# Turning q one tick later in a fused attention and two-MLP kernel, and reordering the last step of its second MLP

## The reference

```
out_d = sm_attn(q_d, k_d, v_d)          # pooled by 4
attn  = softmax(where(|i-j|<4, scale*q@k.T, -1e9))
x     = repeat(out_d, 4) + attn@v       # 2304 x 512
x     = (s*relu(x @ w_in)**2 + b) @ w_out        # 512 -> 2048 -> 512
out   = ((x @ w_a) * (x @ w_b)) @ w_out2         # 512 -> 1536 -> 512
```

## Time and profile before

| | |
|---|---|
| median of three runs | 975.58 us |
| the profiled execution | 975.64 us, of which the span of the trace is 973.8 us |
| PE busy | 951.3 us, 98% of the span |
| ACT, DVE, POOL busy | 474.5, 611.1, 202.0 us |
| granted clock of PE, mean | 0.984 |
| DMA | 71.41 MB, 73 GB/s on average |

### The profile page before, as it was taken

One profiled execution on the slowest core, in us unless ns is written; L12 is line 12 of the kernel. 1 busy time (PEld: TensorE's weight loads), 2 busy tenths in 40 slices (PEclk: granted clock), 3 DMA queues, 4 the chain that ended last, 5 costly groups with the idle time before them and its releaser, 6 DMA issues.

```text
span 973.8 us, 18322 instructions
## 1 busy us (share of the span) xinstructions
PE 951.3 (98%) x6902; PEld 898.5 (92%) x6902; DVE 611.1 (63%) x1087; ACT 474.5 (49%) x1112; POOL 202.0 (21%) x216
## 2 busy tenths in 40 slices
PE   6899999999999999999999999999999999999997
PEld 5799999999999999999999999999999999999996
DVE  5788655655555556555547666666856667766642
ACT  4677554545554445454434544444634345644432
POOL 2200211001210011200012033333333333333310
PEclk8599999999999999999999999999999999999999
DMA  8346220111300122101041142222442222422201
GB/s 199 104 136 164 65 59 20 45 45 43 88 21 20 48 64 67 44 19 44 14 154 34 50 137 66 66 66 66 135 143 79 67 66 66 130 66 65 75 24 66
DMA packets 129352, 71.41 MB, mean 73 GB/s; under 512 B 63248, under 2 KB 120304, under 8 KB 129264
## 3 DMA queue, kind: packets, MB, share of 16 engines
q1 hardware_dynamic: 128224, 69.94, 25.0%
q10 hardware_dynamic: 1040, 0.29, 0.1%
HBM read 60.76 MB, written 9.44 MB: 72 GB/s over the span
## 4 chain that ended last, share of the span: by engine, by line
PE 88%; ACT 6%; DVE 3%; issue 2%; DMA 1%; SPq 1%; POOL 0%; ACTq 0%; DVEq 0%
PE bank L736 27%; PE bank L686 19%; PE bank L672 18%; PE bank L752 15%; ACT sml L795 3%; PE bank L572 2%; PE bank L636 2%; PE bank L619 1%; PE bank L629 1%; PE bank L548 1%; DMA natk<-in_k 1%; ACT smp L786 1%; PE bank L603 1%; PE bank L566 1%; ACT kT L774 1%
## 5 line engine op out<-in xcount | busy, mean ns | idle before, releaser
L736 PE MATMUL bank<-wx 128*128 128x384 f32 x1512 | 287.4, 336 | 0.6 <-ACT u L977 0.6
L736 PEld LDWEIGHTS bank<-wx 128*128 128x128 f32 x1512 | 267.1, 188 | 14.6 <-ACT u L977 0.9
L686 PE MATMUL bank<-g_hi,wx 128*128 128x288 f32 x1024 | 232.1, 302 | 0.0
L672 PE MATMUL bank<-wx 128*128 128x288 f32 x1536 | 226.9, 296 | 0.5 <-ACT relu L889 0.5
L672 PEld LDWEIGHTS bank<-wx 128*128 128x128 f32 x1536 | 211.7, 189 | 0.7 <-ACT relu L889 0.7
L1236 POOL TENSOR_TENSOR raw<-raw 128x256 f32<-128x256 f32 x144 | 143.3, 1013 | 302.9 <-DVE wx L1156 263.4
L686 PEld LDWEIGHTS bank<-g_hi,wx 128*128 128x128 f32 x1024 | 171.4, 188 | 5.3 <-issue 5.2
L752 PE MATMUL bank<-wx 128*128 128x512 f32 x648 | 173.4, 394 | 0.8 <-DVE wx L1156 0.8
L686 PE MATMUL bank<-g_lo,wx 128*128 128x288 f32 x512 | 151.5, 296 | 0.0
L752 PEld LDWEIGHTS bank<-wx 128*128 128x128 f32 x648 | 119.3, 188 | 17.2 <-DVE wx L1156 1.5
L1112 DVE SCALAR_TENSOR_TENSOR g_lo<-relu,b_col,g_hi 128x288 fp32r<-128x288 f32 x128 | 70.6, 552 | 80.4 <-ACT g_hi L894 80.4
(11 more groups left out here) (70 smaller groups left out, 858.8 us busy)
## 6 DMA issues: line engine op xcount, KB each, us to landing
raw<-in_moe_w_b SPq DMA_DIRECT2D x72, 128.0 KB, 2.3
raw<-in_moe_w_a SPq DMA_DIRECT2D x72, 128.0 KB, 2.3
raw<-in_moe_w_out SPq DMA_DIRECT2D x36, 256.0 KB, 2.8
vnat<-in_v SPq DMA_DIRECT2D x32, 144.0 KB
o_transposed<-o_sb SPq DMA_DIRECT2D x8, 576.0 KB, 3.4
o_raw<-o_transposed SPq DMA_DIRECT2D x6, 768.0 KB, 6.3
out<-y SPq DMA_DIRECT2D x18, 256.0 KB, 2.3
natq<-in_q SPq DMA_DIRECT2D x63, 72.0 KB, 2.1
```

Source lines behind the costliest of these rows:

```text
L672: mm = nc.tensor.matmul(HB[:, 0:HALF], wi(w, kd, f), xs(x, c % 2)[:, kd], start=(kd == 0 and j == 0), stop=(kd == KD - 1 and j == 2))
L686: mm = nc.tensor.matmul(ACC[o][:, 0:HALF], wo(w, f, o), g[:, slot % GB, :], start=(f == 0 and j == 0), stop=(f == F1 - 1 and j == 2))
L736: mm = nc.tensor.matmul(dst, left(w, n, a, kd), right(x, i)[:, kd * HC:(kd + 1) * HC], start=(opens and kd == 0 and m == 0), stop=(kd == K ...
```

## The change

Two edits, which share nothing.

1. For units from 4 on, `turn_q`, `take_q` and `sum_q` stand one tick later: -3, -3 and -2 in place of -4, -4 and -3. On PE the three transposes of q move from between up and down of a slot to behind that down, ahead of the next up. On ACT the copy of qT moves from behind relu (L889) to behind the high part of g (L894) and, in the first 16 slots, behind the weight splits (L851). The boot ticks of units 0 to 3 stay.
2. In the last of the 36 steps the products run in the order 0, 1, 2, 4, 5, 3, 6 with the previous step's `down_2` placed anew between them, and DVE has an order of its own: prod0, then c22, then the low part of prod0, then c12, prod1 and its low part.

```diff
--- before.py
+++ after.py
@@ -52,6 +52,10 @@
 N7 = len(PRODUCTS)
 LEFT_AT = {"a11": 0, "a12": 1, "a22": 2, "s1": 3, "s2": 4, "s3": 5, "s4": 6}
 PIECES = 3
+
+SECONDS = (), (0,), (1,), (2, 3), (4, 5), (), ()
+LAST_ORDER = 0, 1, 2, 4, 5, 3, 6
+LAST_SECONDS = (), (0,), (1, 2), (5,), (3, 4), (), ()
 BLK1 = KD * P + DM
 BLK2 = N7 * LEFT + DM
 PIECE = BLK2 // PIECES
@@ -642,7 +646,7 @@
                 for u in at_tick(g, 0, -5, TURN_SKEW):
                     if leads(u):
                         turn_k(u)
-                for u in at_tick(g, 1, -4, TURN_SKEW):
+                for u in at_tick(g, 1, -3, TURN_SKEW):
                     turn_q(u)
                 for u in at_tick(g, 13, 8):
                     if not alone(u):
@@ -757,10 +761,11 @@
                     mm.then_inc(p_used, 1)
 
             for n in range(STEPS):
-                for i in range(N7):
+
+                for i in range(N7) if n < STEPS - 1 else LAST_ORDER:
                     product(n, i)
                     if n > 0:
-                        for tt in ((), (0,), (1,), (2, 3), (4, 5), (), ())[i]:
+                        for tt in (SECONDS if n < STEPS - 1 else LAST_SECONDS)[i]:
                             down_2(n - 1, tt)
             for tt in range(TT):
                 down_2(STEPS - 1, tt)
@@ -972,7 +977,7 @@
                 if over:
                     for tt in range(3):
                         take_y(c - 1, tt)
-                act.wait_ge(up_done, N7 * n + 5)
+                act.wait_ge(up_done, N7 * n + (5 if n < STEPS - 1 else 4))
                 past(act, c22_ready, n)
                 nc.scalar.activation(u3_sb, X_BANK, ACT.Copy).then_inc(u3_taken, 1)
                 if over:
@@ -1075,7 +1080,7 @@
                 for u in at_tick(g, 1, -4, TURN_SKEW):
                     if leads(u):
                         sum_k(u)
-                for u in at_tick(g, 2, -3, TURN_SKEW):
+                for u in at_tick(g, 2, -2, TURN_SKEW):
                     sum_q(u)
 
             def split_w_lo(f):
@@ -1156,6 +1161,23 @@
                 nc.vector.tensor_tensor(p_lo[:, n % 2, h], prod[h], p_hi[:, n % 2, h].bitcast(f32), ALU.subtract)\
                   .then_inc(pl_ready, 1)
 
+            def last_products():
+                n = STEPS - 1
+                dve.wait_ge(up_done, N7 * n + 5)
+                dve.wait_ge(c11_ready, n + 1)
+                nc.vector.tensor_tensor(prod[0], X_BANK, c11_sb, ALU.mult).then_inc(pr1_ready, 1)
+                dve.wait_ge(u3_taken, n + 1)
+                dve.wait_ge(up_done, N7 * n + 6)
+                nc.vector.tensor_tensor(c22_sb, Y_BANK, u3_sb, ALU.add).then_inc(c22_ready, 1)
+                split_product_lo(n, 0)
+                dve.wait_ge(up_done, N7 * n + 7)
+                dve.wait_ge(u2_taken, n + 1)
+                nc.vector.tensor_tensor(c12_sb, Y_BANK, u2_sb, ALU.add).then_inc(c12_ready, 1)
+                dve.wait_ge(c12_ready, n + 1)
+                dve.wait_ge(c22_ready, n + 1)
+                nc.vector.tensor_tensor(prod[1], c12_sb, c22_sb, ALU.mult).then_inc(pr2_ready, 1)
+                split_product_lo(n, 1)
+
             for n in range(STEPS):
                 c, f = divmod(n, F2)
                 renew = f == F2 - 1 and c + 1 < NC2
@@ -1181,6 +1203,9 @@
                     split_w2_lo(n + 2, 1)
                 if 4 <= f < 8 and c + 1 < NC2:
                     right_sum(c + 1, f - 4)
+                if n == STEPS - 1:
+                    last_products()
+                    break
                 dve.wait_ge(u3_taken, n + 1)
                 nc.vector.tensor_tensor(c22_sb, Y_BANK, u3_sb, ALU.add).then_inc(c22_ready, 1)
                 if renew:
@@ -1188,14 +1213,10 @@
                 dve.wait_ge(up_done, N7 * n + 6)
                 dve.wait_ge(c11_ready, n + 1)
                 nc.vector.tensor_tensor(prod[0], X_BANK, c11_sb, ALU.mult).then_inc(pr1_ready, 1)
-
-                if n == STEPS - 1:
-                    split_product_lo(n, 0)
                 dve.wait_ge(up_done, N7 * n + 7)
                 dve.wait_ge(u2_taken, n + 1)
                 nc.vector.tensor_tensor(c12_sb, Y_BANK, u2_sb, ALU.add).then_inc(c12_ready, 1)
-                if n < STEPS - 1:
-                    split_product_lo(n, 0)
+                split_product_lo(n, 0)
                 dve.wait_ge(c12_ready, n + 1)
                 dve.wait_ge(c22_ready, n + 1)
                 nc.vector.tensor_tensor(prod[1], c12_sb, c22_sb, ALU.mult).then_inc(pr2_ready, 1)
```

## The result

The changed kernel takes 986.68 us in the median of four runs (986.18 to 987.52), the kernel before 975.38 (974.59 to 975.60). The profiled execution took 987.52 us, with a span of 985.7 against 973.8.

The account below looks back on a forecast made before the run. PE was taken to bound the kernel, with 88% of the chain. The terms -4.2 + 5.2 + 4.7 + 1.2 + 1.0 - 0.5 = +7.4 us on 975.64 gave 983.0 us, range 980.5 to 985.5.

Parts of the forecast that it names:

- 11 leading units: Units with a k turn: turn_q no longer waits for the copy of kT, 0.38 us each, -4.2 us.
- 12 units without a k turn: From unit 12 on, turn_local waits 0.43 us each for the later copy of q, +5.2 us.
- units 6, 7: ACT's copy of q stands behind two weight splits, so PE waits 2.35 us in each, +4.7 us.
- unit 8: A leading unit whose copy of q also stands behind weight splits; PE waits, +1.2 us.
- the boot's end: Unit 4's later sum of q delays its scores and mask, then unit 5's copy comes later: +1.0 us.
- the last step: c12 starts 0.6 us earlier, product 6 waits 0.14 for c22: -0.5 us.
- what takes the stall's place: turn_local may start 0.94 us behind g_hi's start: leading units wait 0, units without a k turn 0.43 us.
- rival 1: Clock falls at the new stalls, 2.0 us lost per fall: one gives 985.0 us, two 987.0; chance 0.18.
- Rival 2: Copy of q reaches turn_local in time, so 5.2 + 4.7 + 1.2 is not lost: 971.9 us; chance 0.04.

Follow-up runs that it names:

- e6: Changed kernel with unit 4's copy and sum of q back at their old ticks: 985.32 us against 975.74 for the kernel before.
- e7: Kernel before, with q turned, copied and summed later only for the 12 units without a k turn from unit 12 on, plus new last step: 981.11 us.
- e4: Changed kernel with ACT's copy and DVE's sum of q back where they stood, only PE's turn later: 971.44 us against 975.63 for the kernel before.
- e10: Kernel before with only the tick of PE's turn of q changed, old last step: 972.11 us against 975.79.
- e3: Changed kernel with ACT copying q ahead of the two weight splits in the first 16 slots: 978.51 us against 975.63 for the kernel before.
- e1: Kernel before with only the last step's new order: 975.69 us against 975.63.
- e9: Changed kernel with 20, 20 and 15 extra unread matmuls ahead of turn_local for units 6, 7, 8: 983.76 us against 975.79 for the kernel before.
- e2: Kernel before with only q turned, copied and summed one tick later, old last step: 987.14 us against 975.63.
- e8: Kernel before, with q turned, copied and summed later only for units 6, 7 and 8, plus new last step: 983.24 us against 975.74.

## Why the prediction came out as it did

The sign and the places were right; the size was not, because the sum put the clock at nothing: a mechanism that was named and priced, but only as a rival. By the steps of the prediction, in the profiled execution:

```
step                                  forecast   measured   from
11 leading units                        -4.2       -4.0     distances shorter by 0.34 to 0.38
12 units without a k turn               +5.2       +5.2     distances longer by 0.41 to 0.48
units 6, 7                              +4.7       +4.6     2.34, and 18.25 - 15.97 in e6
unit 8                                  +1.2       +1.15    18.26 - 17.11
the boot's end                          +1.0       +1.3     L607 - L603; see below
the last step                           -0.5       -0.3     12.15 to 11.85
falls of the clock                       0         +3.0     two, 1.5 each
second MLP before its last step          -         +0.8     11.31 to 12.15, at chunk changes
sum                                     +7.4      +11.8     span 985.69 - 973.84 = 11.85
```

- **Leading units, and what takes the stall's place: right.** Both distances are 16.4 us, as forecast. e7 shows the loss alone, e4 and e10 the gain alone, and e3 that the weight splits, not transfers, made the long waits of units 6 to 8. The figure for unit 8 is good to some tenths only: its step before, 17.11, held 0.38 us of PE waiting for a transfer of k, and without the edit the same step is 16.88 and 16.90 in e1 and e7.
- **The step that failed is the sum, which has no term for the clock.** "The clock falls at the new stalls" was rival 1, with a chance of 0.18, and the range had room for one fall. Measured are two falls of 1.5 us each, 3.0 in all, out of the 4.4 that the sum is short in the profiled execution. The argument against the fall was one wait of 0.74 us that left the clock full. But the waits forecast were three times as long, and the same trace had a nearer row. Its one fall, at 15.1 us, came behind a stretch with 1.9 us of idle time in 5, and the longest single wait in that stretch was 1.43 us, shorter than the 2.35 that was worked out:

```profile
13.48 0.31 PE L566 MATMUL bank<-pooledk,pooledq 64*72 64x144 f32 x1 [1.43 <-DVE pooledk L994]
```

  The Trainium skill, page "TensorE: Matmul & The Clock Gate", section "HAM oscillation — how this bites in real kernels", has waits between bursts of matmuls send the clock down. I set that aside as not shown by the trace. The page's example has waits of some 3 to 5 us; the falls here stood behind waits of 1.7 to 2.2 us of idle time. e9 shows the mechanism: the same waits with PE kept busy, and no fall.

- **That rival 1's 987.0 is so near the measured 986.68 is in part luck.** Its price per fall was too high, 2.0 for 1.5, since it was taken from the boot's stretch from 41.88 on, 3.9 us, and the stretches here last 3.4. That made up for the 0.8 us in the second MLP, which was not forecast at all. No experiment isolates that term: the chunk change where most of it arises (11.50 us before, 12.23 after) differs between executions of the same code, as shown under e9, and the trace before has the shortest of all.
- **Which of the waits is followed by a fall is not settled.** It is units 6 and 8 in the changed kernel, in e2 and in e8, and unit 7 in e6, with the same three waits each time. The 1.18 us of idle time ahead of unit 5 is followed by no fall in the traces that have it, and neither are the 0.3 of the 12 later units. The traces read give one or two falls, and the times of the changed kernel, of e2 and of e6 spread over 1.3 to 3.0 us. This was not tried further.
- **The boot's end: right in kind, 0.3 too small.** Of the 1.34 us, 0.2 is the later start of this execution. e6 has `turn_pooled` at 50.67, against 51.47 in the changed kernel and 50.13 before, so 0.80 is unit 4's copy and sum, and the 0.35 that is left stays with unit 5's later copy.
- **The last step: right in sign, too large.** Product 6 began behind c22 with PE's pipeline empty, so that c12 came 1.37 behind it, not 1.25, and the wait itself was 0.17, not 0.14.
- **Rival 2** did not happen, but it is what e4 does: with g_hi no longer ahead of the copy the waits are gone. Its number, 971.9, still had the boot's loss in it; e4, without that, is at 971.44.
- **A slip in the working.** The low end for each of units 6 and 7 is given as 2.31. With a handover of 0 it is 65.76 + 0.41 - 63.92 = 2.25, and the +5.0 at the low end of the sum is worked out with that.
